# The fourth pair of heads beside batch 0 goes from a TensorE transpose to a VectorE block transpose with DMAs

## What the kernel computes

```
scores = cap * tanh((q @ k.T / sqrt(D)) / cap)
attn   = exp(scores - max) ; attn /= (sum(attn) + 1e-9)
x      = (attn @ v), heads side by side        # [4*448, 768]
x      = (sigmoid(x @ w_gate) * (x @ w_val)) @ w_out     # 768 -> 1536 -> 768
h      = x @ w_in                              # 768 -> 2048
y      = (h * cos(h)) @ w2_out                 # 2048 -> 768
```

## Time and profile before

| | us |
|---|---|
| median of 3 runs | 1210.38 (1209.56 to 1210.82) |
| the profiled execution | 1210.59 |
| its span in the trace | 1208.8 |
| share of the chain that ended last, TensorE | 95% |
| VectorE, ScalarE, GpSimd busy | 53%, 46%, 49% of the span |
| mean granted clock of TensorE | 0.997 of full speed |

### The profile page before, as it was taken

How to read it: one execution, slowest core, us unless ns; L and a number is a source line. 1 busy time by engine, 2 the same in 40 slices (tenths; PEclk the granted TensorE clock), 3 DMA queues, 4 the chain that set the end, 5 groups by cost and what they waited for, 6 DMA issues and landing times.

```text
span 1208.8 us, 16869 instructions
## 1 busy us (share of the span) xinstructions
PE 1198.7 (99%) x5932; PEld 1090.1 (90%) x5932; DVE 641.2 (53%) x1227; ACT 557.9 (46%) x1053; POOL 594.0 (49%) x542
## 2 busy tenths in 40 slices
PE   8999999999999999999999999999999999999998
PEld 6779999999999989999999999999999999999998
DVE  7951158876763477876651257777662211105610
ACT  8941155656541466666650256766662011105610
POOL 7969968879653356663425416675524100002221
PEclk8999999999999999999999999999999999999999
DMA  4569986776546678788668768787768665666663
GB/s 158 165 240 325 320 305 235 232 236 231 194 160 232 218 249 244 244 250 270 239 227 270 247 199 276 241 254 238 255 226 266 197 222 209 212 222 219 240 233 108
DMA packets 133715, 281.37 MB, mean 233 GB/s; under 512 B 47744, under 2 KB 56704, under 8 KB 133632
## 3 DMA queue, kind: packets, MB, share of 16 engines
q1 hardware_dynamic: 130032, 274.79, 68.2%
q10 hardware_dynamic: 3600, 5.51, 1.2%
HBM read 219.39 MB, written 46.40 MB: 220 GB/s over the span
## 4 chain that ended last, share of the span: by engine, by line
PE 95%; DVE 2%; ACT 1%; issue 1%; DMA 1%; POOL 0%; SPq 0%; ACTq 0%; POOLq 0%
PE acc L877 27%; PE acc L876 27%; PE acc L878 27%; PE s_ps L774 3%; PE s_ps L775 3%; PE acc L829 2%; PE t_ps L846 2%; PE t_ps L848 1%; PE t_ps L811 1%; PE t_ps L795 1%; PE acc L866 1%; PE acc L868 1%; DMA qk_in_whole<-qk 1%; ACT prob L1063 1%; ACT prob L1056 0%
## 5 line engine op out<-in xcount | busy, mean ns | idle before, releaser
L581 POOL TENSOR_SCALAR w_hi<-w_hi_whole 128x768 fp32r<-128x768 f32 (+1 forms) x84 | 77.8, 928 | 348.3 <-DMA w_hi_whole<-w 347.6
L876 PE MATMUL acc<-h_hi,w_hi 128*128 128x448 f32 x672 | 247.4, 368 | 0.0
L877 PE MATMUL acc<-h_lo,w_hi 128*128 128x448 f32 x672 | 245.7, 366 | 0.0
L878 PE MATMUL acc<-h_hi,w_lo 128*128 128x448 f32 x672 | 245.4, 365 | 0.0
L876 PE MATMUL acc<-x_hi,w_hi 128*128 128x448 f32 x576 | 211.0, 366 | 0.0
L877 PE MATMUL acc<-x_lo,w_hi 128*128 128x448 f32 x576 | 210.6, 366 | 0.0
L878 PE MATMUL acc<-x_hi,w_lo 128*128 128x448 f32 x576 | 210.6, 366 | 0.0
L878 PE MATMUL acc<-z_hi,w_lo 128*128 128x448 f32 x384 | 140.2, 365 | 0.0
L876 PE MATMUL acc<-z_hi,w_hi 128*128 128x448 f32 x384 | 140.2, 365 | 0.0
L877 PE MATMUL acc<-z_lo,w_hi 128*128 128x448 f32 x384 | 140.2, 365 | 0.0
L584 POOL TENSOR_TENSOR pt_lo<-pt_lo_whole,pt_hi 128x1344 fp32r<-128x1344 f32 x24 | 74.8, 3116 | 126.0 <-ACT pt_hi L1107 125.9
(11 more groups left out here) (143 smaller groups left out, 2089.1 us busy)
## 6 DMA issues: line engine op xcount, KB each, us to landing
w_lo<-w_pair SPq DMA_DIRECT2D x156, 384.0 KB, 3.8
w_hi<-w_pair SPq DMA_DIRECT2D x108, 384.0 KB, 3.5
w_lo_whole<-w SPq DMA_DIRECT2D x52, 384.0 KB, 3.7
w_pair<-w_lo SPq DMA_DIRECT2D x52, 384.0 KB, 4.3
w_hi_whole<-w SPq DMA_DIRECT2D x48, 384.0 KB, 3.1
w_lo<-w_pair SPq DMA_DIRECT2D x36, 512.0 KB, 4.8
w_hi_whole<-w SPq DMA_DIRECT2D x36, 512.0 KB, 4.0
qk_in_whole<-qk SPq DMA_DIRECT2D x35, 512.0 KB, 6.0
```

Of the source, the lines that this page charges most:

```text
L581: return e.tensor_scalar(out, in_, 1.0, 1.0, ALU.mult, ALU.mult)
L876: e.matmul(out[:, 0:S], w_hi[u % HI][:, wb, :], a_hi[:, kb, :], start=first, stop=False)
L877: e.matmul(out[:, 0:S], w_hi[u % HI][:, wb, :], a_lo[:, kb, :], start=False, stop=False)
L878: return e.matmul(out[:, 0:S], w_lo[u % LO][:, wb, :], a_hi[:, kb, :], start=False, stop=last)
```

## The change

Pair 9 (`EARLY`) joins the pairs that are transposed in blocks. TensorE's transposes of its tiles go, with ScalarE's `pt_high` and VectorE's `pt_low`. VectorE turns its groups 12 and 13 in steps 10 and 11, and groups 14 and 15 between the second and the third product. SyncE issues the 24 DMAs three at a time in eight halves of the third product. ScalarE copies the blocks that stay in units 0 and 1 and rounds in units 3 and 5; VectorE makes the low parts behind units 3 and 5. Pair 9's product with v stays in steps 13 and 15. Other lines adjust counts of semaphores, the order of queries and v of pair 9, and the width of two loads.

```diff
+EARLY = PAIRS + PAIRS // 2
+EARLY_WAYS = 3
+EARLY_FROM = 2 * (U1 + U2) + 7
+    def is_moved(pr):
+        return pr == EARLY or pr >= MOVED
...
+            def move_early(n):
+                per_head = len(WAYS) // EARLY_WAYS
+                d, some = divmod(n - EARLY_FROM, per_head)
+                if not 0 <= d < 2:
+                    return
+                e.wait_ge(s_blocks, moved_no(NG * EARLY + 3) + 1)
+                e.wait_ge(s_pv, 2 * (EARLY - 1) + d + 1)
+                for i, r in WAYS[some * EARLY_WAYS:(some + 1) * EARLY_WAYS]:
+                    e.dma_start(landing(d, i, r), blocks_to(EARLY, d, i, r)).then_inc(s_moved[d], 16)
...
                         if n >= KEEP_LATER:
                             keep(*halves[n - KEEP_LATER])
+                        move_early(n)
...
             def times_v_moved(b, i, d):
...
+                if b == 0:
+                    e.wait_ge(*normalised(tiles_of(group_of(b, NG * i + 3 + d))[-1]))
+                    e.wait_ge(s_g, b * KF2 + KF2 - 1 + d)
...
 +                    if b == 0 and j in (0, 1):
+                        stayed(EARLY, j)
+                    if b == 0 and j in (3, 5):
+                        moved_high(EARLY, j // 2 - 1)
...
 +            def moved_low(pr, d):
+                e.wait_ge(s_pbhi, 2 * moved_idx(pr) + d + 1)
+                at = of_head(d)
+                e.tensor_tensor(pt_lo[:, 0:CH, at], pt_whole[:, 0:CH, at], f32(pt_hi)[:, 0:CH, at],
+                                ALU.subtract).then_inc(s_pblow, 1)
+                e.wait_ge(s_pblow, 2 * moved_idx(pr) + d + 1)
+                e.tensor_tensor(pt_hi[0:D, CH, at], pt_whole[D:P, CH, at], f32(pt_hi)[D:P, CH, at],
+                                ALU.subtract).then_inc(s_pb, 1)
...
             def attend(b, n):
...
+                if b == 0 and group_of(b, n + 2) in (NG * EARLY, NG * EARLY + 1):
+                    turn_blocks(group_of(b, n + 2))
...
                     normalise(group_of(b, last), zeros[0])
+                    for g in (NG * EARLY + 2, NG * EARLY + 3):
+                        turn_blocks(g)
                     row_max(group_of(b, last + 1))
...
             def third_product(b):
...
                         e.tensor_tensor(h_lo[:, 2 * j + h, :], acc[2 * p + h][:, 0:S], f32(h_hi)[:, 2 * j + h, :], ALU.subtract).then_inc(s_g, 1)
+                    if b == 0 and j in (3, 5):
+                        moved_low(EARLY, j // 2 - 1)
```

More of the change, by code:

```diff
@@ L210, in build, with moved_idx, with_gap @@
     s_out = [sem(f"y_stored{p}") for p in range(2)]
+    def is_moved(pr):
+        return pr == EARLY or pr >= MOVED
+    def moved_idx(pr):
+        return 0 if pr == EARLY else pr - MOVED + 1
+    def with_gap(pr):
+        return is_moved(pr) or pr == EARLY + 2
     K_AT = (0, S + GAP)
@@ L219, in queries @@
     def queries(pr, d, of=qk_in):
-        return of[pr % 2][d][:, 0:S + GAP] if d else of[pr % 2][d][:, KW:KW + S + (GAP if pr >= MOVED else 0)]
+        return of[pr % 2][d][:, 0:S + GAP] if d else of[pr % 2][d][:, KW:KW + S + (GAP if with_gap(pr) else 0)]
     def turned(pr, t):
-        return t > MID if pr < ALONE else pr < MOVED and t in [ts[1] for ts in GROUPS if len(ts) > 1]
+        return t > MID if pr < ALONE else not is_moved(pr) and t in [ts[1] for ts in GROUPS if len(ts) > 1]
     def keys_of(pr, t):
@@ L330, in moved_no, with split_count, transposed_count @@
     def moved_no(g):
-        return g - NG * MOVED
+        return NG * moved_idx(g // NG) + g % NG
+    def split_count(x):
+        early = range(TILES * EARLY, TILES * (EARLY + 1))
+        return min(x, early[0] - 1) - TILES * ALONE + 1 if x <= early[-1] else x - TILES * (ALONE + 1) + 1
+    def transposed_count(x):
+        return TILES * ALONE + split_count(x) if x >= TILES * ALONE else x + 1
     def prob_of(g):
@@ L338, in prob_of @@
             return last_prob if ts[0] == TILES - 1 else prob[:, ts[0]:ts[-1] + 1, :]
-        at = moved_no(g) % 3 * 2
+        at = (g - NG * MOVED) % 3 * 2
         return prob[:, at:at + len(ts), :]
     def turned_by_tensor(b, n):
-        return 0 <= n < STEPS and group_of(b, n) < NG * MOVED
+        return 0 <= n < STEPS and not is_moved(group_of(b, n) // NG)
     def turned_blocks(pr, d):
@@ L406, in load_qk @@
                     e.wait_ge(s_score, NG * (pr - 2) + (NG if d else 2))
-                at = slice(0, QK if d or pr >= MOVED else KW + S)
+                at = slice(0, QK if d or with_gap(pr) else KW + S)
                 if (pr, d) == (0, 0):
@@ L928, in attend @@
                 if i >= 0 and r in (1, 3):
-                    if pair_of(b, i) < MOVED:
+                    if not is_moved(pair_of(b, i)):
                         times_v(b, i, r // 2)
@@ L1332, in turn_blocks @@
                 e.wait_ge(*normalised(tiles_of(g)[-1]))
[L1333 to L1336, removed]
+                if part in (0, 2) and pr > EARLY:
+                    e.wait_ge(s_moved[d], 16 * len(WAYS) * moved_idx(pr))
+                    e.wait_ge(s_stayed, 4 * (2 * (moved_idx(pr) - 1) + d + 1))
                 if d == 0 and pr % PAIRS in (0, BESIDE_H):
@@ L1586 @@
     q_b = np.concatenate([q_t[1][:, :, :LAST], gap, q_t[1][:, :, LAST:]], axis=2)
+    moved = [EARLY] + list(range(MOVED, heads // 2))
     for q_d, of, first in ((q_a, q_t[0], 0), (q_b, q_t[1], QB // 2)):
-        by_quarters = of[MOVED:].reshape(-1, D, 4, QUARTER)
+        by_quarters = of[moved].reshape(-1, D, 4, QUARTER)
         last = slice(QUARTER - QB // 2, QUARTER) if first == 0 else slice(0, QB // 2)
         whole = slice(0, QUARTER - QB // 2) if first == 0 else slice(QB // 2, QUARTER)
-        q_d[MOVED:] = 0.0
-        q_d[MOVED:, :, :LAST] = by_quarters[..., whole].reshape(-1, D, 4, MID, QB).transpose(0, 1, 3, 2, 4).reshape(-1, D, LAST)
-        q_d[MOVED:, :, LAST:].reshape(-1, D, 4, QB)[..., first:first + QB // 2] = by_quarters[..., last]
+        q_m = np.zeros_like(q_d[moved])
+        q_m[:, :, :LAST] = by_quarters[..., whole].reshape(-1, D, 4, MID, QB).transpose(0, 1, 3, 2, 4).reshape(-1, D, LAST)
+        q_m[:, :, LAST:].reshape(-1, D, 4, QB)[..., first:first + QB // 2] = by_quarters[..., last]
+        q_d[moved] = q_m
     of_a = np.concatenate([k_a, q_a], axis=2)
```

58 lines of the change are left out of this document (32 added, 26 removed).

## The result

| | before | changed |
|---|---|---|
| median, in turns on one chip, 8 runs each | 1210.64 us (1209.56 to 1212.13) | 1214.36 us (1213.62 to 1215.76) |
| the profiled execution, its span | 1210.59, 1208.8 | 1214.61, 1212.8 |
| mean granted clock of TensorE | 0.997 | 0.997 |

The ratio is 1.0031, 95% interval 1.0020 to 1.0042: 3.7 us slower. The forecast was 1213.1. Three of the four predicted waits stand where they were expected and in that order, the fourth (0.34 us, at unit 3) is not there, and two losses that are not waits were not foreseen: a stretch at half clock and a slower pace of the matmuls. Timelines come from one profiled execution of a kernel, times from the median of its runs.

What follows compares the result with a forecast made beforehand. TensorE, busy for 1198.7 of 1208.8 us, was taken to bound the kernel. -3.05 + 1.06 + 0.34 + 1.34 + 3.02 = +2.7 us gave 1213.1 us, range 1208.5 to 1215.5 with the rivals (its own 1211.5 to 1215).

Steps and rivals of the forecast that it cites:

- the four predicted waits: TensorE's waits: 1.06 us for `z_low`, 0.34 at unit 3, 1.34 before unit 6, 3.0 before the fourth product.
- What goes: Second and fourth products: 25 transposes and a bank wait leave TensorE, 3.05 us, of which 0.76 and 2.29.
- VectorE ahead of `z_low`: End of the second product: added turns start `z_low` at 248.8, not 247.80, and TensorE waits 1.06 us.
- The chain of a unit: Third product: unit 0 ready without a wait, unit 1 ready at 268.9 but wanted at 268.6, a wait of 0.34 us.
- The meetings: Behind units 3 and 5: VectorE's two `moved_low` instructions wait for GpSimd and take 4.0 and 4.8 us.
- Unit 6 and the fourth product: TensorE waits 1.34 us before unit 6 and 3.0 us at the start of the fourth product.
- The numbers around the sum: The main case's chance 0.64 and range 1211.5 to 1215, split into 0.44 slower and 0.20 same.
- DMAs and queues: SyncE's issues, landings, wider loads and GpSimd's extra splitting: margins suffice, cost 0, at most 1 us.
- (a): Low parts cost VectorE only 2.2 us, so only waits of 1.06 and 0.34 remain: -1.65, 1208.7; chance 0.19.
- (b): Everything is hidden, the 1.06 us wait for `z_low` included: -3.05, 1207.3; chance 0.07.
- (c): A queue falls behind, a landing or split weight late for ScalarE or TensorE by 2 to 4 us: 1216; chance 0.07.
- (d): The change does not do what it says, transposes left or TensorE's waits moved elsewhere: same as before; chance 0.03.

Runs made afterwards that it cites:

- e5: Changed kernel with group 13 turned behind `z_low`, groups 14 and 15 between unit 0's halves, and copies, rounding and low parts respread; 1208.23 us, -2.3 against the kernel before.
- e3: Changed kernel with the turn of group 13 moved behind `z_low` and `x_low`, nothing left out; 1214.25 us, +3.3 over the kernel before, ratio 1.0020.
- e1: Changed kernel with the second operand of both low-part instructions read from one repeated PSUM bank column; 1209.58 us, -1.4 against the kernel before, ratio 0.9990.
- e8: Changed kernel without VectorE's semaphore wait between the two low-part instructions; 1213.70 us, +3.2 over the kernel before, ratio 1.0028.
- e2: Changed kernel with both low-part instructions eight columns wide, TensorE multiplying the high part instead of the low; 1209.49 us, -1.5 against the kernel before, ratio 0.9987.
- e10: Kernel before with ten small VectorE reductions ahead of the last `z_low` of batch 0; 1211.69 us, +1.0 over the kernel before, ratio 1.0007.
- e6: Changed kernel with group 13 turned behind `z_low` and the second head's low parts in the fourth product; 1209.89 us, ratio 1.0001 to the kernel before.
- e7b: Changed kernel with ten 128-column `ident` matmuls ahead of the wait before the fourth product; 1212.19 us, +1.5 over the kernel before, ratio 1.0010.
- e4: Changed kernel with only the second head's low parts moved behind step 13 of the fourth product; 1210.49 us, -0.5 against the kernel before, ratio 0.9993.
- e7: Changed kernel with twenty 128-column `ident` matmuls ahead of the wait before the fourth product; 1213.96 us, +3.4 over the kernel before, ratio 1.0032.

## Why the prediction held, and where it did not

**What goes.** Right. The transposes gave back 0.75 us in the second product and about 2.26 in the fourth, by the account above; e5, where no wait takes their place, is 2.3 us below the kernel before (1.3 to 3.5).

**VectorE ahead of `z_low`.** Right: 248.65 against 248.8, a wait of 0.81 against 1.06. The difference is the step from the releasing instruction's start to the matmul: 0.88 by my reading of the earlier trace rows, and 0.68 here (248.65 to 249.33). It is 0.71 before the fourth product too, and 0.2 too much in each of my waits. `z_low` came 0.15 before its time, but so did TensorE.

**The chain of a unit.** I gave 0.34 us at unit 3, and there was none: `h_lo` of unit 1 starts at 267.53, so with 0.71 it is there at 268.24, not at 268.9, while TensorE came at 268.65, as counted (268.6). The chain by hand ran 0.6 us too late at units 0 and 1. That the slack is thin holds: in e3, with unit 0 later, unit 2 waits 0.67.

**The meetings.** The step on which the sign hung was right: 4.0 and 4.8 us predicted, 4.18 and 4.66 measured. The split between the two instructions was not: I gave the first over 2 us, and it took 1.96 and 1.89, while the second took 2.15 and 2.71. e1 is the strongest evidence, since it keeps the widths and the place and moves one operand (which is then also one repeated column); that GpSimd's own instruction shrinks from 3.02 to 1.84 in it says that the two engines held each other up. The Trainium skill (SBUF — State Buffer, "Who interferes with whom") says that the loser of such a meeting blocks fully, and the trace agrees: GpSimd's 1.85 became 3.02 and VectorE's 0.62 (e1) became 2.15. One point of my reasoning was wrong: I had let GpSimd slip in "at the semaphore", and e8, without the semaphore, shows the same 2.15.

**Unit 6 and the fourth product.** 0.93 measured for 1.34, and 2.47 for 3.02. Both include the 0.2 of the release. The remainder is that unit 6's first low part began at 308.32, while by my chain it was 308.9.

**What was missing.** The sum had no term for the clock. I had taken a wait at its length, and the longest of them cost 2.47 + 1.65. No row of the kernel before shows a wait of that length in a busy stretch, so it could not be read from there; a bound would have been right. The second missing term, the pace, is 0.8 us, and 0.2 stands behind the first two waits. That the forecast came within 1.3 us is partly luck: my four waits were 1.55 us too large in sum (0.25, 0.34, 0.41 and 0.55), and what I left out, 2.65 us, was more than that. With the clock's 1.65 alone added, the forecast would have been 1214.8, near the measured 1214.4 only because the remaining errors nearly cancel.

**The numbers around the sum.** Two do not follow from it. With the meetings between 6.2 and 10.2 us and a us of time for each, the sum runs from 1210.5 to 1214.5, not from 1211.5 to 1215. And three quarters of 0.64 are 0.48, where I wrote 0.44; spread evenly between the sum's own bounds, less than half of it lies above 1212.8.

**DMAs and queues.** No cost, as forecast. ScalarE has no wait on a landing in the profile, and e1 and e5 keep all the DMAs: e5 is faster than the kernel before, and e1 is at least no slower (its interval ends at 1.0000).

**The rivals.** (a) was the time of e1, -1.4 against -1.65 given, but not of this kernel. (b) did not happen here; e5, with the work placed otherwise, comes within 0.75 us of it. (c) was not seen. (d) is out: the changed kernel has no transpose of TensorE between 237 and 331 us.

**Left open.** Where the pace of 0.2067 us comes from. It need not belong to the change: it turns up where the products are those of the kernel before. In e1's profiled execution it fills the third products of batches 1 and 2 as well,

```profile
552.15 0.37 PE L914 MATMUL acc<-z_hi,w_lo 128*128 128x448 f32 x1
...
589.35 0.37 PE L914 MATMUL acc<-z_hi,w_lo 128*128 128x448 f32 x1
```

180 matmuls in 37.20 us again (36.48 at this place in the kernel before, in e2 and in e10), and in e3's it runs from 82 to 157 us in the first product of batch 0, which takes 94.58 us there and 93.08 in the kernel before. In the third product of batch 0 it shows in nine of the eleven profiled executions of the changed kernel and its variants (not in e3 and e5, and for only 7 us in e6), and in neither the kernel before nor e10; so a link with the change is possible, but not shown. It is not the wait for `z_low` alone (e10, e7b), not GpSimd's delay (e1 and e2 have it too), and not the order of the instructions alone: e7b is the same program as the changed kernel up to 306 us, but there the pace changes only in the seventh half, where both profiles of the changed kernel have it from the second. It ended at the wait before unit 6 in those three and lasted to the end of the stage in e1, e2, e4, e7 and e8.

Nor is it settled what length of standing still makes the clock fall: it fell after 2.47 and 2.48 us (the changed kernel twice, and e3), and did not after 2.17 (e8). A second wait of that kind stands in batch 1 of e4's profiled execution, 2.10 us long, and the granted clock behind it is 1.00:

```profile
552.86 0.47 PE L912 MATMUL acc<-z_hi,w_hi 128*128 128x448 f32 x1 [1.94 <-DVE z_lo L1494]
```

## What to carry to other kernels

Work that moves from the bounding engine to others needs slack in the chain that feeds that engine, at the very places where it is put; here the same instructions, placed elsewhere (e5), turned +3.7 us into -2.3. Before putting a two-input SBUF instruction on VectorE beside a busy GpSimd, price it at its own time plus up to one of GpSimd's instructions each (here 0.4 for the first and 1.5 to 2.1 for the second), or see whether one operand can lie in a bank. And take the longest wait of TensorE in a busy stretch out first: here the one of 2.47 us cost 4.1, while those of about 1 us cost their length and 0.1.

## What was not expected of the hardware

- **An idle time costs clock behind it.** After 2.47 us of standing, the granted clock was at half for a good 3 us and cost 1.65 more (0.60 over 309.0 to 313.3); ten useless matmuls in the gap kept it at 1.00 and saved 1.9 us of the whole. The waits of 0.81, 0.93 and 1.11 us showed none, nor did those of 2.10 (e4) and 2.17 (e8).
- **GpSimd's turn.** A waiting GpSimd instruction gets in between two VectorE instructions issued back to back (2.15 us for one of 0.62), semaphore or not; one that was not yet waiting did not (0.16 us for 64x8, twice in e2).
- **Two paces at one clock.** Matmuls of 448 columns went at 0.2027 or 0.2067 us each over tens of us, with a granted clock of 1.00 in both, also where the program is the same (e1 and e2 in batch 1).
- **A matmul of `ident` by `ident`, 128 columns, float32, took 0.219 us**, twice the 0.109 of a transpose of 128 columns; the trace has 40 records for 20 of them (e7).
